# Small constant tensors allocated ahead of the large SBUF tensors instead of behind them (fused attention and two feed-forward stages, fp32, one core)

## The reference

```python
qn = q / (norm(q, axis=1) + 1e-6);  kn = k / (norm(k, axis=1) + 1e-6)   # [1, 6016, 256]
s = kn.transpose(0, 2, 1) @ qn / tau                                      # [256, 256]
a = exp(s - s.max(-1));  a /= a.sum(-1) + 1e-9
x = (v @ a).reshape(6016, 256)
xn = x / sqrt(mean(x * x, -1) + 1e-6) * rms_g
g = xn @ w_gate
x = ((g / (1 + exp(-g))) * (xn @ w_val)) @ w_out                          # 256 -> 1536 -> 256
h = x @ w_in2
out = (h - tanh(h)) @ w_out2                                              # 256 -> 2048 -> 256
```

## Time and profile before

| | |
|---|---|
| median of three runs | 1245.73 us (1245.35 to 1246.84) |
| the profiled execution, its own time | 1246.84 us |
| its span, first to last instruction | 1245.0 us |
| TensorE (PE) busy | 1212.4 us, 97% |
| TensorE weight loads (PEld) | 1021.8 us, 82% |
| VectorE (DVE) busy | 860.3 us, 69% |
| ScalarE (ACT) busy | 377.1 us, 30% |
| GpSimd (POOL) busy | 68.1 us, 5% |
| mean granted TensorE clock | 0.994 |

### The profile page before, as it was taken

How to read it: one execution, slowest core, us unless ns; L and a number is a source line. 1 busy time by engine, 2 the same in 40 slices (tenths; PEclk the granted TensorE clock), 3 DMA queues, 4 the chain that set the end, 5 groups by cost and what they waited for, 6 DMA issues and landing times.

```text
span 1245.0 us, 16669 instructions
## 1 busy us (share of the span) xinstructions
PE 1212.4 (97%) x5715; PEld 1021.8 (82%) x5715; DVE 860.3 (69%) x1390; ACT 377.1 (30%) x645; POOL 68.1 (5%) x38
## 2 busy tenths in 40 slices
PE   6789999999999999999999999999999999999998
PEld 5678888888888888888888888888888888888876
DVE  7978965766766766667676676576676676666665
ACT  6553421421421331321322232242142132132121
POOL 5533300000000000000000000000000000000000
PEclk9889999999999999999999999999999999999999
DMA  7633000000000000000000000000000000000000
GB/s 266 222 125 119 1 13 18 1 1 35 1 0 34 0 0 34 0 0 34 0 1 17 17 0 17 17 0 17 17 0 0 34 0 0 17 0 0 18 1 18
DMA packets 16875, 33.91 MB, mean 27 GB/s; under 512 B 1872, under 2 KB 8528, under 8 KB 16848
## 3 DMA queue, kind: packets, MB, share of 16 engines
q1 hardware_dynamic: 16704, 33.30, 7.8%
q10 hardware_dynamic: 144, 0.26, 0.1%
HBM read 27.40 MB, written 6.16 MB: 27 GB/s over the span
## 4 chain that ended last, share of the span: by engine, by line
PE 91%; DVE 5%; issue 2%; ACT 1%; DMA 0%; SPq 0%; DVEq 0%; ACTq 0%
PE ring L801 50%; PE out_acc L814 20%; PE y_acc L814 15%; PE ring L763 3%; DVE out_rows L527 2%; DVE h_hi L660 1%; PE ring L786 1%; PE ring L747 1%; PE ring L774 1%; DMA qk_in<-in_q_dram 0%; PE y_acc L726 0%; DVE act L693 0%; DVE act L671 0%; DVE qk_lo L522 0%; PE y_acc L731 0%
## 5 line engine op out<-in xcount | busy, mean ns | idle before, releaser
L477 ACT ACTIVATE act<-ring 128x512 f32<-128x512 f32 (+1 forms) x336 | 198.4, 590 | 687.5 <-PE ring L801 684.2
L662 DVE TENSOR_TENSOR h_lo<-act,h_hi 128x512 fp32r<-128x512 f32 (+1 forms) x336 | 233.4, 695 | 11.6
L801 PE MATMUL ring<-x_hi,we_hi 128*128 128x512 f32 (+1 forms) x576 | 225.2, 391 | 4.7 <-DVE act L671 3.4
L801 PE MATMUL ring<-x_hi,we_lo 128*128 128x512 f32 (+1 forms) x576 | 222.8, 387 | 0.0
L801 PE MATMUL ring<-x_lo,we_hi 128*128 128x512 f32 (+1 forms) x576 | 222.8, 387 | 0.0
L671 DVE TENSOR_TENSOR act<-ring,act 128x512 f32<-128x512 f32 (+1 forms) x144 | 97.9, 680 | 168.6 <-ACT act L477 168.4
L693 DVE TENSOR_TENSOR act<-ring,act 128x512 f32<-128x512 f32 (+1 forms) x192 | 130.1, 678 | 97.5 <-ACT act L477 96.5
L660 DVE CAST h_hi<-act 128x512 fp32r<-128x512 f32 (+1 forms) x336 | 157.1, 468 | 13.9
L814 PE MATMUL out_acc<-h_hi,wl_hi 128*128 128x512 f32 (+1 forms) x384 | 148.2, 386 | 2.3 <-DVE h_lo L662 2.3
L801 PE MATMUL ring<-y_hi,wl_hi 128*128 128x512 f32 (+1 forms) x384 | 148.9, 388 | 1.2 <-DVE y_lo L683 0.9
L801 PE MATMUL ring<-y_hi,wl_lo 128*128 128x512 f32 (+1 forms) x384 | 147.9, 385 | 0.0
(11 more groups left out here) (100 smaller groups left out, 1266.2 us busy)
## 6 DMA issues: line engine op xcount, KB each, us to landing
qk_in<-in_k_dram SPq DMA_DIRECT2D x15, 384.0 KB, 3.8
qk_in<-in_q_dram SPq DMA_DIRECT2D x15, 384.0 KB, 4.7
v_in<-in_v_dram SPq DMA_DIRECT2D x11, 512.0 KB, 3.3
out_dram<-out_rows SPq DMA_DIRECT2D x10, 512.0 KB, 2.6
w_in<-in_moe_w_out_dram SPq DMA_DIRECT2D x14, 256.0 KB, 3.1
w_in<-in_moe_w_in_dram SPq DMA_DIRECT2D x8, 256.0 KB, 3.2
w_in<-in_moe_w_gate_dram SPq DMA_DIRECT2D x6, 256.0 KB, 4.0
w_in<-in_moe_w_val_dram SPq DMA_DIRECT2D x6, 256.0 KB, 4.8
```

Source lines behind the costliest of these rows:

```text
L477: nc.scalar.activation(act[:, u % RING, 0:width], b.bank(name)[:, 0:width], func).then_inc(act_ready, 1)
L662: nc.vector.tensor_tensor(h_lo[:, slot, 0:width], act[:, slot, 0:width], f32(h_hi[:, slot, 0:width]), ALU.subtract).then_inc(h_ready, 1)
L801: ins = nc.tensor.matmul(b.bank(name)[:, 0:width], weights(c, w_part), (hi if part else lo)[:, c, 0:width], start=c == 0 and w_part and pa ...
```

## The change

The fifteen small tensors keep their names, sizes and uses, but are allocated earlier: four behind `ones`, three behind `x_lo`, eight behind `we_lo`. Nothing else is edited. The order of instructions, their operands, sizes and waits is the same on every engine in both kernels, and the lines behind the allocations move up by one.

```diff
         ident = sb("ident", [P, P], F32)
         ones = sb("ones", [P, P], F32)
+        eps = sb("eps", [P, 1], F32)
+        tau_c = sb("tau_c", [P, 1], F32)
+        rtau = sb("rtau", [P, 1], F32)
+        g_c = sb("g_c", [P, KC], F32)
         a_hi = sb("a_hi", [P, KC, C], F32R)
...
         x_lo = sb("x_lo", [P, KC, TILE], F32R)
+        ssq = sb("ssq", [P, TILE // P], F32)
+        rms = sb("rms", [P, TILE // P], F32)
+        rrms = sb("rrms", [P, TILE // P], F32)
         act = sb("act", [P, RING, TILE], F32)
...
         we_lo = sb("we_lo", [P, EARLY, BLOCK], F32R)
+        norms = sb("norms", [P, 2 * KC], F32)
+        rnorms = sb("rnorms", [P, 2 * KC], F32)
+        rk = sb("rk", [P, KC], F32)
+        warm = sb("warm", [P, 1], F32)
+        top = sb("top", [P, KC], F32)
+        ntop = sb("ntop", [P, KC], F32)
+        total = sb("total", [P, KC], F32)
+        rtotal = sb("rtotal", [P, KC], F32)
...
         wl_lo = sb("wl_lo", [P, BLOCKS - EARLY, BLOCK], F32R)
-
-        eps = sb("eps", [P, 1], F32)
...
-        rtotal = sb("rtotal", [P, KC], F32)
```

## The result

The changed kernel took 1258.49 us (1258.27 to 1259.54, 4 runs), the kernel before 1246.13 us beside it. The ratio is 1.0101, 95% interval 1.0087 to 1.0115. I had forecast 1245.8 us within 1243.0 to 1257.0, with no change as the likeliest case. That was wrong in kind, and the time lies 1.5 us above the range.

A forecast was written before the change was run, and what follows sets the result against it. The prediction took TensorE's pace to bound about 1115 us, with DMA, VectorE and TensorE sharing the first 130 us. Its terms summed to 0 against 1246.84 us profiled, given as 1245.8 us for a median, range 1243.0 to 1257.0.

The forecast's parts named there:

- What bounds the kernel: TensorE's pace for about 1115 us; in the first 130 us DMA, VectorE and TensorE hand work to each other.
- The large tensors: New start addresses of TensorE's moving operands: taken as 0, between +10.6 and -5.8 us.
- Weights as the stationary operand: All of `we` and `wl` move to 96 modulo 256; taken as 0, as loads are covered unless they grow 20%.
- The 38 ns of cover: A weight load takes 189 ns under a matmul pace of 226.7 ns, which leaves each load this margin.
- The upper bound of 8 columns, 3.3 ns,: Per matmul, up to 32 more bytes fetched for an off-boundary moving operand; 10.6 us over 3168 matmuls with y or h moving.
- Rival A: L801 with `y` moving and L814: TensorE pays at a misaligned moving operand's edge; 10.6 us slower, 1256.4 us; chance 0.14.
- Rival C: L801 with `x` moving: starts at multiples of 256 help; 5.8 us faster, about 1240 us; chance 0.12.
- VectorE, ScalarE: In the tiles, `act`, `h`, `y` and `out` go to 96 modulo 256; taken as 0, any growth lying beside TensorE.
- the start-up: First 130 us and first tile, VectorE work and q and k loads without cover: taken as 0, within -1 and +5.
- the small tensors: `eps`, `g_c`, `rrms` and the rest start at multiples of 32 bytes: taken as 0, less than 0.2 us either way.
- Rival B: Start-up: VectorE's two-input instructions or q and k loads slow down; 4.1 or 4.8 us, about 1250 us; chance 0.17.
- The rule of 16-byte lines: SBUF is read in 16-byte lines, only crossing to a new one penalised; each operand covers as many lines, time unchanged.

The follow-up runs named there:

- e1: Kernel before with one unused 32-byte tensor behind `ones`, so every large tensor starts 32 bytes later; 1245.87 us, ratio 0.9999.
- e2: Kernel before with one unused 96-byte tensor between `x_lo` and `act`, so the weights and everything else behind x move; 1259.60 us, ratio 1.0109.
- e3: Changed kernel with one unused 160-byte tensor behind `rrms`, so `act` and all behind it start at 0 modulo 256, like x; 1246.70 us, ratio 0.9997.
- e4: Kernel before with one unused 96-byte tensor between `w_in` and `we_hi`, so all weights move and x, h, y stay; 1278.58 us, ratio 1.0257.
- g1: Kernel before with padding so that only the low weights, `we_lo` and `wl_lo`, start 96 bytes further modulo 256; 1271.79 us, ratio 1.0209.

## Why the prediction was wrong

- **What bounds the kernel** held: TensorE has no slack in the tiles, so a pace wider by 7 ns came out in full.
- **The large tensors** is the step that failed. I took each operand's start alone and put its cost at 0, with +10.6 us as a bound. The three groups shift by 128, 224 and 480 bytes, and the differences between them, 96 and 256, were in my own table; I never asked whether TensorE's two operands matter to each other. e1 shows that a common shift of 32 bytes costs nothing, e2 and e3 that the difference of 96 is the whole loss of 12.4 us.
- **Weights as the stationary operand** failed with it. The 38 ns of cover is real and the load's record grew by 2 ns only, yet moving the weights alone (e4) cost 32 us. Cover speaks of a longer load; the pace widened with loads about as long as before.
- **The upper bound of 8 columns, 3.3 ns,** was too small: the pace grew by 6.7 ns. It was no bound, since it assumed a mechanism (bytes fetched at an edge) that no row supported. The range's upper end rested on it.
- **Rival A** came to 1256.4 us, close in size and wrong in everything else: it had y and h pay and x keep its pace, and it is the other way round; that the time came near its price, and near the range's end, is luck. Its condition had a slip too: half a nanosecond in 3168 matmuls is 1.6 us, and the 2.5 us belongs to 0.8 ns. **Rival C**, x better off at 256, had the sign of that stretch wrong.
- **VectorE, ScalarE, the start-up and the small tensors** at nothing were right: 692, 427 and 599 ns, 52.88 us of TensorE work in the first 70, and q and k landing in 4.7 and 3.8 us as before. Rival B is out. (VectorE would bound the tiles when it grows by the 48% of its cover, not by a third.)
- The rule of 16-byte lines that I cited from the Trainium skill (Advanced Engine Details and Errata, "Memory Cachelines") fits e1 (ratio 0.9999). It doesn't carry the conclusion that I drew from it, an unchanged time: all starts here are multiples of 16, and a difference of 32 costs 28.7 us. The measurement decides.

What stays open: why unequal remainders slow TensorE. That the weights' load meets the stream of another matmul in SBUF is my guess; e4's trace shows that the load starts with the current matmul and that no other engine is needed, but g1 couldn't separate a matmul's own pair from its neighbour's. Open too are the asymmetry (64 against 192), and why 384 columns pay nothing in e4 and up to 3 ns at 128 and 160 bytes and in the changed kernel. No run made the 256-column products unequal, and none used another type than fp32r.

## What to carry to other kernels

Where fp32r matmuls of 512 columns bound a kernel, as here, keep the moving operand and the weights at the same remainder modulo 256 bytes: allocate small tensors behind the large ones, or pad each group of small ones to 256 bytes, which costs nothing (e3). When a change moves addresses, list the differences between the starts of tensors that are read at the same time, not only the starts. And read TensorE's pace from the chain's counted stretches: the loss of 1% is plain there and nearly absent from loads and from the busy shares.

## What the hardware showed that I hadn't expected

- 512-column fp32r matmuls pace at about 227 ns with equal remainders, and at 228.9 to 234.2 ns with offsets of 32 to 192 bytes; an offset of 256 bytes is free.
- 384-column matmuls with h moving take 173.3 ns both at 0 and, in e4, at an offset of 96 (4.16 us for 24), and 176.3 to 176.7 ns at 128 and 160 (4.23 and 4.24 us).
- The slower pace outlasts its cause: by three matmuls in the changed kernel, and in the kernel before five wide distances follow the 256-column products. One unequal pass in three slows the whole stretch by more than its share.
- VectorE's and ScalarE's 512-column instructions in the tiles take the same time within 1 ns (692 or 693, 427, 599 or 600) at starts of 0, 32 or 96 modulo 128.
